# Ten middle token tiles of an attention and two-stage MoE kernel, written out instead of looped over

## The chip, the cores and the metric

The kernel runs on one core of one Trainium2 chip. The metric is the device time of one execution in microseconds, lower is better.

## What is computed

Three stages follow each other, all in float32. Cut to what matters:

```python
def _attn_ref(q, k, v):                        # 8 batches, 8 heads, 576 tokens, head size 64
    scores = scale * np.matmul(q_c, k_c.transpose(0, 1, 2, 4, 3))   # within chunks of 64 tokens
    attn = np.exp(scores - scores.max(-1)); attn /= attn.sum(-1) + 1e-09
    out = np.matmul(attn, v_c)
def _moe_ref(x, w_in, w_out, s, b):            # x 4608 x 512, hidden 2048
    r = np.maximum(x @ w_in, 0.0)
    g = s * (r * r) + b
    return g @ w_out
def _moe2_ref(x, w_skip, w_gate, w1, w2):      # 8 experts, hidden 1024, one expert per token
    do_compute = x @ w_skip > 0
    e_idx = np.argmax(xc @ w_gate, axis=1)     # xc = x[do_compute]
    h = np.maximum(xc[mask] @ w1[e], 0.0)      # mask: e_idx == e
    y[mask] = gate_w[mask, None] * (h @ w2[e])
    out[do_compute] = xc + y
```

## The kernel before, in words

**Tiles.** The 4608 tokens are cut into 12 tiles of 384 tokens (`TILES`, `TOK`), a tile into 6 attention chunks of 64 tokens (`CPT`). The hidden layer of the first MoE is cut into 16 slices of 128 (`FT`). Every float32 product is made of three products of high and low parts (`_hi`, `_lo`).

**Two phases.** The first 960 us or so go over the 12 tiles: while TensorE does the first MoE of tile i, all engines also do the attention of tile i+1 and the routing of tile i-1. Then come the experts, in blocks of 128 gathered rows, in loops whose bounds are known only at run time.

**What a tile is on TensorE** (`tile`, L756 to L780): for each of the 16 slices f, `into_h` of slice f+1 (L714, matmuls on L723, 12 of 384 columns) and then `into_x2` of slice f (L728, matmuls on L738, 9 of 512 columns); between them stand the attention stages of tile i+1 that `stages(f)` names (L688, L695, L704) and, in slice 14, `rank` of the tile before (L749 to L753). The last slice calls `into_h(i + 1, 0, ...)`, so the first slice of the next tile is computed before the tile ends. That call waits for `x_ready`, which VectorE gives on L1140 when the last attention chunk is in. At the end of a tile TensorE waits for `route_step` (L778).

**The other engines** have a `tile` of the same shape. ScalarE (L997): `relu` (L985), square (L989), the high part of g (L916) and its share of the attention. VectorE (L1253): the low part of g (L1186), `keep_x2` of the tile before at slice 0 (L1196), the gate's dot products (L1207), `route_a` and `route_b` (L1246 to L1251 are its last steps, which need `rank`). GpSimd (L580): low parts of q, k and v and, behind each tile, `send_records` (L563). SyncE loads and stores in a loop of its own, one tile an iteration (L451).

**What sets the order.** The order is written out by hand, in the sequence of calls on each engine; engines meet at counting semaphores. Tile 0 and tile 11 are straight code (L807, L811). Tiles 1 to 10 are a loop of five iterations with two tiles in each, on TensorE (L808), ScalarE (L1028), VectorE (L1296) and GpSimd (L607). The two tiles of an iteration differ in the buffer z (1, then 0). Inside the loop the tile's number is held in a register, so a wait for a count such as `CPT * i + end // CHUNK` is preceded by register operations; in straight code it is a constant. An iteration's end is a compare-and-branch back to its start. TensorE's is:

```python
            tile(0, 0, True, False)
            with pe.Fori(0, (TILES - 2) // 2) as two:
                tile(two * 2 + 1, 1, True, True)
                tile(two * 2 + 2, 0, True, True)
            tile(TILES - 1, 1, False, True)
```

Of the kernel before, what the change touches and what calls it, by code (L numbers as in the profile page):

```python
# [17 lines left out]
def chunked_attention_moe(nc, first_qk_rows, first_v_rows, qk, v, w_in, w_out, moe_s, moe_b, gate_rows, gate_cols_in, w1, w2, out):  # L18
    CHUNK = 64
    D = 64  # L20
    N, DM = out.shape
    FF = w_in.shape[0] * w_in.shape[2] // (DM // P)
    E, _, F = w1.shape
    KT = DM // P
    FT = FF // P
# [4 lines left out]
    TILES = N // TOK  # L30
# [41 lines left out]
    with ctx:  # L72
# [244 lines left out]
        def stages(f):  # L317

            found = []
            for c in range(CPT):  # L320
                for name, at in (("D", 2 * c + 4), ("C", 2 * c + 3), ("B", 2 * c + 1), ("A", max(2 * c - 1, 0))):
                    if at == f:
                        found.append((name, c))
            return found
# [192 lines left out]
        def _(pool):  # L517
# [23 lines left out]
            def lo_of_qk(n, c):  # L541

                pool.wait_ge(qk_hi, n - CPT + 1)
                pool.tensor_tensor(qk_rest[:, :], qk_raw[:, c % SLOTS, :], qk_top[:, :].bitcast(F32),  # L544
                                   ALU.subtract).then_inc(qk_split, 1)

            def lo_of_v(n):

                pool.wait_ge(v_hi_done, n - CPT + 1)
                pool.tensor_tensor(v_lo[:, :], v_raw[:, :], v_hi[:, :].bitcast(F32), ALU.subtract).then_inc(v_split, 1)  # L550
# [7 lines left out]
            def send_records(i):  # L558

                pool.wait_ge(table_clear, 16)  # L560
                pool.wait_ge(records_ready, i + 1)
                for t in range(SUB):
                    pool.indirect_dma_start(  # L563
                        out=table[:, :], out_offset=bass.IndirectOffsetOnAxis(ap=slot[:, t:t + 1].bitcast(U32), axis=0),
                        in_=record[:, t, :], in_offset=None, bounds_check=E * REGION - 1,
                        oob_is_err=False).then_inc(records_out, 16)
# [13 lines left out]
            def tile(i):  # L580
                for f in range(1, FT):
                    for stage, c in stages(f - 1):
                        if stage == "A":
                            lo_of_qk(CPT * (i + 1) + c, c)
                        if stage == "C":
                            lo_of_v(CPT * (i + 1) + c)
                    if isinstance(i, int) and i == 0 and f % 2 and f + 2 < JOBS:
                        column_sums(f + 2)
# [15 lines left out]
                    split_half(step - 2)  # L604
            column_sums(1)
            tile(0)
            with pool.Fori(1, TILES - 1, 2) as odd:  # L607
                for i in (odd, odd + 1):
                    tile(i)
                    send_records(i - 1)  # L610
            def gather(count, stored):

                pool.wait_ge(x2_stored, 32 * stored)
# [33 lines left out]
        def _(pe):  # L647
# [108 lines left out]
            def tile(i, z, attend, route):  # L756

                for f in range(FT):
                    if attend and f == 2 * CPT + 2:
                        into_h(i, f + 1, z, range(1))  # L760
                        attention("D", CPT * (i + 1) + CPT - 1, CPT - 1)
                        into_h(i, f + 1, z, range(1, KT))
                    elif f + 1 < FT:
                        into_h(i, f + 1, z, begin=0 if route or f > 0 else FIRST_PART)
                    elif attend:
                        into_h(i + 1, 0, 1 - z)
                    if route and f == RANK_AT[attend]:
                        if attend:
                            pe.wait_ge(probs_kept, CPT * (i + 1) + CPT)
                        rank(i - 1)  # L770
                    if attend and f != 2 * CPT + 2:
                        for stage, c in stages(f):
                            attention(stage, CPT * (i + 1) + c, c)
                    if not route and f == FT - 1:
                        column_sums()
                    into_x2(i, f)
                if route and attend:
                    pe.wait_ge(route_step, ROUTE_STEPS * (i - 1) + RANKS_READ)  # L778
                if not route:
                    pe.wait_ge(bias_done, 1)  # L780

            def column_sums():

                pe.wait_ge(column_step, JOBS - 1)
                pe.wait_ge(exp_done, 2 * CPT)
                pe.matmul(s_ps[:, :], products[:, 0:P], bias[:, :], start=True, stop=True).then_inc(sums_done, 1)
# [18 lines left out]
            into_h(0, 1, 0, range(KT // 2, KT), end=FIRST_PART)  # L805
            into_h(0, 0, 0, begin=FIRST_PART)
            tile(0, 0, True, False)  # L807
            with pe.Fori(0, (TILES - 2) // 2) as two:  # L808
                tile(two * 2 + 1, 1, True, True)
                tile(two * 2 + 2, 0, True, True)  # L810
            tile(TILES - 1, 1, False, True)  # L811

            ht_ps = [s_ps, av_ps]
# [100 lines left out]
        def _(act):  # L914
# [82 lines left out]
            def tile(i, z, attend, route):  # L997
                for f in range(FT):
                    relu(i, f)
                    waiting = stages(f - 1) if attend and f > 0 else []  # L1000
                    order = {1: "AgCDB", FT - 1: "DgCAB"}.get(f, "CgADB")
                    for name in order:
                        if name == "g":
                            hi_of_g(i, f)
                        for stage, c in waiting:
                            if stage == name:
                                attention(stage, CPT * (i + 1) + c, c, 1 - z, i + 1)
                    if route and f == RANK_AT[attend]:
                        route_exp(i - 1)
                    if not route and EARLY + f < JOBS:  # L1010
                        split(EARLY + f)
                    for e, j in jobs_at(f) if not attend else ():
                        split2(e, 1 - e, j)
# [11 lines left out]
            act.wait_ge(scalars_in, 32)  # L1025
            act.wait_ge(sums_done, 1)
            act.activation(bias[:, :], s_ps[:, :], ACT.Identity, scale=b_col[:, 0:1]).then_inc(bias_done, 1)
            with act.Fori(0, (TILES - 2) // 2) as two:  # L1028
                tile(two * 2 + 1, 1, True, True)
                tile(two * 2 + 2, 0, True, True)  # L1030
            tile(TILES - 1, 1, False, True)
            ht_ps = [s_ps, av_ps]

# [77 lines left out]
        def _(dve):  # L1111
# [141 lines left out]
            def tile(i, z, attend, route):  # L1253
                for f in range(FT):
                    waiting = stages(f - 1) if attend and f > 0 else []
                    order = "DCBg" if f == FT - 1 else "CBgD"
                    for name in order:
                        if name == "g":
                            lo_of_g(i, f)
                        for stage, c in waiting:  # L1260
                            if stage == name:
                                attention(stage, CPT * (i + 1) + c, c, 1 - z)
                    if route and f == 0:
                        keep_x2(i - 1)
                    if route and f < RANK_AT[attend]:
                        dots(i - 1, DOTS_BY[attend][f], DOTS_BY[attend][f + 1])
                    for stage, c in waiting:
                        if stage == "B":
                            attention("B2", CPT * (i + 1) + c, c, 1 - z)
                    if route and f == RANK_AT[attend] - 1:  # L1270
                        route_a(i - 1)
                    if route and f == RANK_AT[attend]:
                        route_b(i - 1)
                    if not attend and f == RANK_AT[attend]:
                        dve.wait_ge(route_step, ROUTE_STEPS * i)
                        for e in range(SOON):
                            es = next_row[:, e:e + 1]
                            dve.tensor_scalar(es, es, float(e * REGION + P), None, ALU.max).then_inc(first_closed, 1)
                        dve.wait_ge(first_closed, SOON)
                    if not route and EARLY + f < JOBS:  # L1280
                        split(EARLY + f)
                    for e, j in jobs_at(f) if not attend else ():
                        split2(e, 1 - e, j)
                    if not attend and f == FT - 4:
                        dve.wait_ge(got_in, 16)
                        dve.tensor_copy(idx[:, :], got[:, :]).then_inc(rows_held, 16)
# [6 lines left out]
            tile(0, 0, True, False)  # L1293
            dve.wait_ge(bias_done, 1)
            dve.wait_ge(gate_in, 16)
            with dve.Fori(0, (TILES - 2) // 2) as two:  # L1296
                tile(two * 2 + 1, 1, True, True)
                tile(two * 2 + 2, 0, True, True)
            tile(TILES - 1, 1, False, True)
            keep_x2(TILES - 1)  # L1300

# [181 lines left out]
```

## Time and profile before

| | |
|---|---|
| median of 3 runs | 1352.35 us (1352.3 to 1354.8) |
| the profiled execution's own time | 1355.16 us |
| its span in the trace | 1353.4 us |
| mean granted TensorE clock | 0.997 of full speed |
| instructions with a busy time | 22395 |

The profiled execution lies 2.8 us above the median, and its span is 1.8 us shorter than its own time. Times in the trace count from the first instruction of the span. PE is TensorE's matmuls, PEld its weight loads, DVE VectorE, ACT ScalarE, POOL GpSimd; a name ending in q (PEldq, DVEq) is that engine's sequencer, whose instructions are not counted as busy. "Idle before" is time in which the engine had nothing running, with what ended it; "issue" means that the profile shows nothing that it waited for.

### The profile page before, as it was taken

To read this page: it belongs to the slowest core of one execution; us is meant where nothing else is said; L and a number is where in the kernel's file an instruction comes from. 1 tells how busy PE (TensorE), PEld (TensorE's weight loads), DVE (VectorE), ACT (ScalarE), POOL (GpSimd) and SP (SyncE) were. 2 spreads that over 40 slices of the span, in tenths; PEclk is the share of its full clock that TensorE was granted. 3 is DMA by queue.
4 is the path that set the end of the run, shared out by engine and by line. 5 is a ranking of instruction groups with operands and counts; after the bars stand their busy time and mean duration, and the time that the engine had idled before them with its cause. 6 is when DMAs were issued, how large, how long until landed. Compare 5 with 4: busy or idle time off the path is not lost.

```text
span 1353.4 us, 22395 instructions
## 1 busy us (share of the span) xinstructions
PE 1329.0 (98%) x7066; PEld 1171.8 (87%) x7067; DVE 927.9 (69%) x2141; ACT 753.0 (56%) x1838; POOL 311.1 (23%) x274
## 2 busy tenths in 40 slices
PE   8999999999999999999999999999998999999998
PEld 7998999899998999889998999988786778888886
DVE  3887869688786978778796878867548673333232
ACT  4886757576674757567575766646346552222221
POOL 4642223121322212221322222101111111111111
PEclk9999999999999999999999999999899999999999
DMA  7531202031121302112030302044618641111110
GB/s 261 171 116 58 98 29 98 22 103 39 44 93 30 100 30 99 32 50 88 32 106 22 106 24 91 23 141 127 218 59 296 226 146 47 39 47 39 46 38 27
DMA packets 61589, 116.95 MB, mean 86 GB/s; under 512 B 11848, under 2 KB 20296, under 8 KB 61360
## 3 DMA queue, kind: packets, MB, share of 16 engines
q1 hardware_dynamic: 44496, 81.11, 18.0%
q10 hardware_dynamic: 10880, 20.97, 4.4%
q0 software_dynamic: 6112, 13.56, 3.2%
q8 instruction: 58, 0.95, 0.3%
q14 instruction: 43, 0.35, 0.1%
HBM read 91.28 MB, written 27.08 MB: 87 GB/s over the span
## 4 chain that ended last, share of the span: by engine, by line
PE 90%; DVE 5%; issue 3%; ACT 1%; DVEq 1%; POOLq 0%; POOL 0%; ACTq 0%
PE h_ps L723 29%; PE y_ps L738 28%; PE y_ps L848 10%; PE h_ps L834 10%; PE s_ps L688 3%; PE av_ps L704 3%; DVE weights_lo L1180 2%; PE t_ps L695 1%; PE s_ps L842 1%; PE t_ps L820 1%; PE av_ps L842 1%; PE h_ps L651 0%; DVE rows_t_lo L1313 0%; DVE weights_lo L1171 0%; DVE g_lo L1186 0%
## 5 line engine op out<-in xcount | busy, mean ns | idle before, releaser
L1207 DVE CUSTOM_DVE_ANT_0 products<-scratch,wide 128x512 f32<-128x512 f32 x297 | 287.3, 967 | 6.7
L723 PE MATMUL h_ps<-rows_t_hi,weights_lo 128*128 128x384 f32 (+2 forms) x776 | 262.1, 338 | 7.8 <-issue 5.6
L723 PE MATMUL h_ps<-rows_t_hi,weights_hi 128*128 128x384 f32 (+2 forms) x776 | 260.9, 336 | 0.0
L723 PE MATMUL h_ps<-rows_t_lo,weights_hi 128*128 128x384 f32 (+2 forms) x776 | 259.7, 335 | 0.0
L985 ACT ACTIVATE scratch<-h_ps 128x384 f32<-128x384 f32 x192 | 94.5, 492 | 294.5 <-PE h_ps L723 289.8
L738 PE MATMUL y_ps<-weights_hi,g_lo 128*128 128x512 f32 x576 | 228.1, 396 | 1.6 <-DVE g_lo L1186 1.6
L738 PE MATMUL y_ps<-weights_lo,g_hi 128*128 128x512 f32 x576 | 226.5, 393 | 0.0
L738 PE MATMUL y_ps<-weights_hi,g_hi 128*128 128x512 f32 x576 | 225.9, 392 | 0.0
L1186 DVE TENSOR_TENSOR g_lo<-scratch,g_hi 128x384 fp32r<-128x384 f32 x192 | 120.1, 626 | 91.7 <-ACT g_hi L916 89.2
L723 PEld LDWEIGHTS h_ps<-rows_t_hi,weights_lo 128*128 128x128 f32 x776 | 145.8, 188 | 21.5 <-issue 7.3
L544 POOL TENSOR_TENSOR qk_lo<-qk_raw,qk_hi 128x768 fp32r<-128x768 f32 x66 | 125.3, 1899 | 141.6 <-ACT qk_hi L916 141.6
L723 PEld LDWEIGHTS h_ps<-rows_t_lo,weights_hi 128*128 128x128 f32 x776 | 145.8, 188 | 7.0
L550 POOL TENSOR_TENSOR v_lo<-v_raw,v_hi 128x256 fp32r<-128x256 f32 x66 | 49.1, 744 | 436.3 <-ACT v_hi L916 436.3
L723 PEld LDWEIGHTS h_ps<-rows_t_hi,weights_hi 128*128 128x128 f32 x776 | 145.6, 188 | 0.0
L738 PEld LDWEIGHTS y_ps<-weights_hi,g_hi 128*128 128x128 f32 x576 | 108.1, 188 | 23.7
L738 PEld LDWEIGHTS y_ps<-weights_hi,g_lo 128*128 128x128 f32 x576 | 108.2, 188 | 20.5 <-DVE g_lo L1186 2.7
L738 PEld LDWEIGHTS y_ps<-weights_lo,g_hi 128*128 128x128 f32 x576 | 108.2, 188 | 17.0 <-issue 0.2
L933 ACT ACTIVATE soft<-s_ps,row_bias 64x64 f32<-64x64 f32 x528 | 120.4, 303 | 3.0
L916 ACT ACTIVATE rows_t_hi<-av_ps 64x256 fp32r<-64x256 f32 (+2 forms) x165 | 68.2, 413 | 67.5 <-PE av_ps L842 58.9
L916 ACT ACTIVATE g_hi<-scratch 128x384 fp32r<-128x384 f32 x192 | 100.8, 525 | 6.1
L848 PE MATMUL y_ps<-weights_hi,rows_t_lo 128*128 128x512 f32 x240 | 97.2, 405 | 6.1 <-DVE rows_t_lo L1313 5.7
L834 PE MATMUL h_ps<-weights_hi,rows_t_lo 128*128 128x512 f32 x244 | 102.1, 418 | 0.0
(178 smaller groups left out, 2377.1 us busy)
## 6 DMA issues: line engine op xcount, KB each, us to landing
qk_raw<-in_qk SPq DMA_DIRECT2D x66, 384.0 KB, 3.0
expert_raw<-in_w ACTq DMA_DIRECT2D x25, 512.0 KB, 5.4
expert_raw<-in_w SPq DMA_DIRECT2D x21, 512.0 KB, 5.4
out<-scratch SPq DMA_DIRECT2D x12, 768.0 KB
x_rows<-scratch SPq DMA_DIRECT2D x12, 768.0 KB
v_raw<-in_v SPq DMA_DIRECT2D x66, 128.0 KB, 2.0
scratch<-in_w ACTq DMA_DIRECT2D x15, 512.0 KB
wide<-in_w_out SPq DMA_DIRECT2D x7, 512.0 KB, 4.5
```

The source lines that it names most:

```text
L544: pool.tensor_tensor(qk_rest[:, :], qk_raw[:, c % SLOTS, :], qk_top[:, :].bitcast(F32), ALU.subtract).then_inc(qk_split, 1)
L550: pool.tensor_tensor(v_lo[:, :], v_raw[:, :], v_hi[:, :].bitcast(F32), ALU.subtract).then_inc(v_split, 1)
L688: mm = pe.matmul(s_ps[:, J * 256:(J + 1) * 256], qt[:, J, :], kt[:, J, :], start=m == 0, stop=m == 2)
L723: mm = pe.matmul(h_ps[f % 2][:, begin:end], w[:, f // PAIR, kt, fs], x[:, z, kt, begin:end], start=kt == 0 and n == 0, stop=kt == KT - 1 a ...
L738: mm = pe.matmul(y_ps[t][:, :], g[:, f % 2, ts], w[:, f, :], start=f == 0 and n == 0, stop=f == FT - 1 and n == 2)
L834: mm = pe.matmul(h_ps[f][:, :], x[:, kt, :], w[par][:, f, kt, :], start=kt == 0 and n == 0, stop=kt == KT - 1 and n == 2)
L848: mm = pe.matmul(y_ps[0][:, :], h[:, t, :], w[par][:, t, :], start=t == 0 and n == 0, stop=t == ET - 1 and n == 2)
L916: return act.activation(out_, in_, ACT.Copy)
L933: last = act.activation(probs[xs, c % 2, h, :], s_blocks[xs, h, x, :], ACT.Exp, bias=row_bias[xs, h:h + 1], scale=SCALE)
L985: act.activation(r_buf[f % 2], h_ps[f % 2][:, 0:TOK], ACT.Relu).then_inc(r_done, 1)
L1186: dve.tensor_tensor(GL[:, f % 2, :], u_buf[f % 2], GH[:, f % 2, :].bitcast(F32), ALU.subtract).then_inc(g_ready, 1)
L1207: dve.tensor_tensor_reduce(products[:, :], x2_sb[:, t, :], gate_w[:, e, :], 1.0, 0.0, ALU.mult, ALU.add, logits[:, t, e:e + 1]).then_inc(d ...
```

## The change

On TensorE, ScalarE, VectorE and GpSimd the loop over pairs of tiles is replaced by a Python loop, which writes tiles 1 to 10 out one behind the other. The tile's number is then a constant in every wait. SyncE's loop over tiles, the work of a tile and its order are as before.

```diff
@@ GpSimd, L607 @@
             tile(0)
-            with pool.Fori(1, TILES - 1, 2) as odd:
-                for i in (odd, odd + 1):
-                    tile(i)
-                    send_records(i - 1)
+            for i in range(1, TILES - 1):
+                tile(i)
+                send_records(i - 1)
@@ TensorE L808; the same edit on ScalarE L1028 and VectorE L1296 @@
             tile(0, 0, True, False)
-            with pe.Fori(0, (TILES - 2) // 2) as two:
-                tile(two * 2 + 1, 1, True, True)
-                tile(two * 2 + 2, 0, True, True)
+            for i in range(1, TILES - 1):
+                tile(i, i % 2, True, True)
             tile(TILES - 1, 1, False, True)
```

## Rows read from the trace of the kernel before

**Rows 1.** The page: busy time by engine, and the chain that ended last.
```profile
PE 1329.0 (98%) x7066; PEld 1171.8 (87%) x7067; DVE 927.9 (69%) x2141; ACT 753.0 (56%) x1838; POOL 311.1 (23%) x274
...
PE 90%; DVE 5%; issue 3%; ACT 1%; DVEq 1%; POOLq 0%; POOL 0%; ACTq 0%
```

**Rows 2.** Waits, 109 to 891 us: waiter <- awaited: total us, times, longest.
```profile
PEld h_ps L723 <- issue: 7.3, 4, 2.3
...
PE h_ps L723 <- issue: 5.6, 4, 1.9
PE h_ps L723 <- DVE rows_t_lo L1140: 1.7, 5, 0.3
```

**Rows 3.** Stretches, one a tile (1, 2, 3, 4, 6, 8, 10): us, busy, clock, DMA.
```profile
109.19:186.44 77.25, 77.25 (x430) 70.34 (x430) 63.16 (x152) 50.87 (x140) 19.20 (x15) 1.00 0.19 62
186.44:265.19 78.75, 77.22 (x430) 70.13 (x429) 63.76 (x154) 50.32 (x139) 18.71 (x15) 1.00 0.19 62
265.19:342.64 77.45, 77.45 (x430) 70.71 (x431) 61.40 (x150) 50.31 (x139) 18.71 (x15) 1.00 0.19 62
342.64:421.56 78.92, 77.24 (x430) 70.15 (x429) 63.89 (x154) 50.31 (x139) 18.71 (x15) 1.00 0.19 61
...
499.01:578.54 79.53, 77.26 (x429) 70.17 (x429) 64.48 (x155) 50.32 (x139) 18.71 (x15) 1.00 0.19 61
...
656.00:734.69 78.69, 77.22 (x430) 70.13 (x429) 63.67 (x154) 50.32 (x139) 18.71 (x15) 1.00 0.19 61
...
812.11:889.67 77.56, 77.23 (x430) 70.47 (x430) 62.57 (x152) 50.32 (x139) 18.72 (x15) 1.00 0.15 50
sum 780.48, PE 773.18 PEld 704.21 DVE 626.30 ACT 503.70 POOL 187.58; mean PE 77.32 PEld 70.42 DVE 62.63 ACT 50.37 POOL 18.76
```

**Rows 4.** The chain, 255 to 275 us: start us, us, what.
```profile
259.55 2.35 PE h_ps L723 x12
261.90 2.09 PE y_ps L738 x9
263.99 1.21 issue
265.19 2.32 PE h_ps L723 x12
```

**Rows 5.** The chain, 184 to 190 us and 882 to 895 us.
```profile
186.44 2.10 PE h_ps L723 x12
...
889.67 2.10 PE h_ps L723 x12
```

**Rows 6.** Branches of loops, by line: ns min/median/max.
```profile
L808 PEldq COMPARE_BRANCH  x5: 83/4738/5475, 260.3 to 886.0; - x5
...
L1296 DVEq COMPARE_BRANCH  x5: 60/68/72, 259.2 to 884.9; - x5
...
L900 PEldq COMPARE_BRANCH  x20: 67/208/214, 1060.0 to 1332.3; - x20
```

**Rows 7.** DMA queues, 109 to 891 us, then 260.5 to 266.5 us: packets, MB.
```profile
q8 instruction: 43, 0.70, 0.5%
...
q8 instruction: 2, 0.03, 4.6%
```

**Rows 8.** Timeline, PE and DVE, tiles 1, 2 and 11: rank's end, next step.
```profile
179.63 0.22 PE L753 MATMUL t_ps<-chosen,ones 128*128 128x8 bf16 x3
...
179.96 0.18 DVE L1246 TENSOR_TENSOR place<-t_ps,next_row 128x24 f32<-128x24 f32 x1 [1.44 <-PE t_ps L753]
...
256.85 0.22 PE L753 MATMUL t_ps<-chosen,ones 128*128 128x8 bf16 x3
...
257.52 0.18 DVE L1246 TENSOR_TENSOR place<-t_ps,next_row 128x24 f32<-128x24 f32 x1 [1.80 <-PE t_ps L753]
...
929.47 0.22 PE L753 MATMUL t_ps<-chosen,ones 128*128 128x8 bf16 x3
...
929.79 0.18 DVE L1246 TENSOR_TENSOR place<-t_ps,next_row 128x24 f32<-128x24 f32 x1 [1.51 <-PE t_ps L753]
```

**Rows 9.** Timeline, DVE, first work behind the loop's end, tile 3.
```profile
263.58 0.56 DVE L1186 TENSOR_TENSOR g_lo<-scratch,g_hi 128x384 fp32r<-128x384 f32 x1 [3.49 <-ACT g_hi L916]
264.17 1.41 DVE L1196 SCALAR_TENSOR_TENSOR scratch<-y_ps,s_col,bias 128x512 f32<-128x512 f32 x2
```

More of the change, by code:

```diff
@@ L1027, in _ @@
             act.activation(bias[:, :], s_ps[:, :], ACT.Identity, scale=b_col[:, 0:1]).then_inc(bias_done, 1)
-            with act.Fori(0, (TILES - 2) // 2) as two:
-                tile(two * 2 + 1, 1, True, True)
-                tile(two * 2 + 2, 0, True, True)
+            for i in range(1, TILES - 1):
+                tile(i, i % 2, True, True)
             tile(TILES - 1, 1, False, True)
@@ L1295, in _ @@
             dve.wait_ge(gate_in, 16)
-            with dve.Fori(0, (TILES - 2) // 2) as two:
-                tile(two * 2 + 1, 1, True, True)
-                tile(two * 2 + 2, 0, True, True)
+            for i in range(1, TILES - 1):
+                tile(i, i % 2, True, True)
             tile(TILES - 1, 1, False, True)
```

## The prediction

> **What bounds the kernel now.** Read the page first: TensorE's matmuls are busy for 1329.0 us, 98% of the span, and the chain that ended last runs on PE for 90% of it [rows 1]. With no matmul taken away, a change can win only what PE is idle or late, so the next view is the waits of PE in the part that the change touches, 109 to 891 us. What PE waited for there is short to tell: four times "issue", 5.6 us in all, which is PE waiting for nothing that another engine owes it, and five times VectorE's L1140, 1.7 us; the weight loads show the same four stops as 7.3 us [rows 2]. Four is the number of jumps back in a loop of five iterations, five is the number of second tiles.
>
> Then the stretches: I cut the loop at the start of each tile's `into_h(i, 1)`, which gives a duration per tile [rows 3]. The first tile of a pair takes 77.25 us (tile 1) or 77.45 us (tile 3), the second 78.69 to 79.53 us when a jump back follows and 77.56 us in tile 10, where none does. The granted clock is 1.00 in all of them. So the cost is at a place, not spread.
>
> The chain shows that place: behind the 9 matmuls of the last slice (261.90 us) come 1.21 us of issue, then `into_h(3, 1)` at 265.19 us, whose 12 matmuls take 2.32 us [rows 4]. The same 12 at the boundary inside a pair take 2.10 us and follow without a gap, as they do at the loop's exit [rows 5]: same work, no jump. The sequencer's own rows name the cause: TensorE's branch on L808 has a median of 4.7 us and a maximum of 5.5 us, and a minimum of 83 ns, the one not taken [rows 6]. It is issued some 3.7 us ahead of the last matmul (from 260.3 us, against an end at 263.99 us), which is why only part of it shows. Between 260.5 and 266.5 us the queue that carries instructions moved two blocks of 16 KB, where 43 in 782 us is the mean of one in 18 us [rows 7]: I read it as fetching the loop's start anew. The loops of the expert phase jump in 0.2 us [rows 6], so it is not a jump as such, but a jump to code that is no longer held.
>
> **The change, part by part.** All durations are of the profiled execution (1355.16 us, span 1353.4); it is 2.8 us above the median of 1352.35. The terms are differences inside it, and I take them off the median.
>
> *The four jumps back on TensorE go.* Ends of second tiles: 78.75 + 78.92 + 79.53 + 78.69 = 315.89 us, against 4 x 77.56 = 310.24 us of the tile without a jump: 5.65 us. The first matmuls behind a jump refill the pipeline (2.32 against 2.10 us), which stands in the odd tiles: all ten sum to 780.48 us, the even ones to 315.89 + 77.56 = 393.45, the odd ones to 387.03, against 5 x 77.25 = 386.25: 0.78 us. Together **6.43 us**. This sum agrees with the 5.6 us of waits and 4 x 0.2 of refill.
>
> *The late step of VectorE in second tiles.* The second tile without a jump (77.56) is 0.31 us longer than the first (77.25). The timeline says where: in tile 1 `rank` ends at 179.63 + 0.22 = 179.85 us and VectorE's L1246 starts 0.11 us later; in tile 2 it ends at 257.07 and L1246 starts 0.45 us later; in tile 11, which is straight code, 0.10 us later [rows 8]. Behind L1246 stand L1140 and `x_ready`, for which PE's `into_h(i + 1, 0)` waits; that is the 1.7 us in five times [rows 2]. The code of both tiles is the same but for constants and the register arithmetic, so the 0.34 us is tied to the position in the instruction stream or to the registers; written out, neither is repeated five times at that spot. I take 5 x 0.31 = **1.55 us**. Bounds: nothing, if it comes back at other tiles' L1246, or 1.55 us lost more (ten times instead of five).
>
> *Register operations before waits go* on all four engines. On PE they stand beside matmuls that run anyway: in tiles 1 and 3 the PE is busy for the whole stretch, 77.25 of 77.25 and 77.45 of 77.45 us [rows 3]. On VectorE and ScalarE they could shorten the path to `x_ready`: the 12 matmuls behind it take 2.35 us in tile 2 [rows 4] against 2.10, so at most about 0.25 us in each of 10 tiles, 2.5 us, could be won. I take 0, because L1246 to L1251 are paced by their own results, and keep the 2.5 us for the low end.
>
> *The jumps on VectorE, ScalarE and GpSimd go.* VectorE's takes 0.07 us [rows 6] and its next work is 3.49 us later, waiting for ScalarE's g_hi [rows 9]; GpSimd is busy 23% of the span. Worth 0: ScalarE's own jump is hidden by the same wait for PE's h.
>
> *What is late next, where the stall goes.* PE will ask for `into_x2(3, 0)` 1.2 us earlier, and that needs g_lo and the y banks that `keep_x2` frees from 264.17 us on, 1.41 us for two of them [rows 9]. Without the stall `into_h(3, 1)` ends at 263.99 + 2.10 = 266.1 us, g_lo is done at 264.14 and the second bank at 265.58 (for 266.1 + 0.7). The cover holds, by at least 1 us, and the boundary inside a pair has the same order with no gap. SyncE's loop is not changed; DMA is at 0.19 in these stretches, and its loads follow PE's progress.
>
> *The longer code.* The number of executed instructions falls a little, so the fetches of 16 KB stay about 43 less the extra ones. In straight sequence they cost PE nothing: of 43 fetches between 109 and 891 us only those at the four jumps have a wait beside them [rows 2, 7]. The nearest row for a fetch that would not be hidden is the jump's 1.2 to 1.9 us.
>
> Sum: 6.43 + 1.55 = 7.98 us, all on the path that sets the end. What follows (tile 11 and the experts) is the same code started earlier: 1352.35 - 8.0 = **1344.4 us**, 0.6% faster.
>
> One page of the Trainium skill speaks against this. "Advanced Engine Details and Errata", section Control Flow Timing, gives a compare-and-branch about 108 ns; by that figure four jumps would be worth an estimated 0.4 us and nothing would be measured. The branches that are not taken or short agree with it (83 ns and 68 ns), the 4.7 us of L808 do not, and the measurement decides.
>
> **The rivals.**
> - *The late step stays or moves* (chance 0.15). Only the jumps' 6.43 us go: 1345.9 us. If L1246 is late in all ten tiles, 1.55 us more are lost: 1347.5 us. For it: the cause of the 0.34 us is not in any row. Against: tile 11.
> - *The jump was not the cause, the boundary is* (0.03). If PE needs a refill of instructions at this point whatever stands there, the four stops stay, and the time is within 1 us of 1352.35. Against: two kinds of boundary without jump and without gap [rows 5].
> - *Fetches fall behind in straight code: slower* (0.03). TensorE's ten tiles become some 35 blocks never run before, where each must arrive in its turn. The place is PE's wait "issue" in mid-tile. It decides from 8.0 / 35 = 0.23 us a block; at the 0.5 us that would be a part of the jump's stop, it is 35 x 0.5 - 8.0 = 9.5 us slower, 1361.9 us. Against: tiles 0 and 11 and 30-odd blocks inside the loop show none.
> - *A loop of the experts loses its quick jump* (0.05). Their code moves to other addresses. If a jump of 0.2 us on L900 becomes one of 4.7, hidden for the most part as at L808, it costs about 1.4 us each time; once or twice, 1345.8 to 1347.2 us; in all 20, 28 us, which would be slower by 20. For the latter nothing speaks: these loops are short.
>
> **How the numbers follow.** The forecast has 0.74. A difference of under 0.2%, 2.7 us, can't be told from no change in this kernel, so "faster" means under 1349.6 us. Forecast, late step and most of the experts' case lie below it: 0.94. No change 0.03, slower 0.03. The range: from 1344.4 less the 2.5 us of the register operations, 1341.9, a little lower for the runs' scatter, to 1347.5 of the first rival and a little more: 1341.5 to 1348.5 us.
>
> **What would show it.** In the profile after: no wait "PE h_ps <- issue"; ten stretches of about 77.25 us, summing to about 772.5 instead of 780.5; no branch on TensorE before the experts; L1246 0.10 us behind `rank` in each tile; no cluster of 16 KB blocks at the former jumps. Wrong would be: a new PE wait in mid-tile, a second tile still 0.3 us longer (first rival), or an expert phase (from the first matmul of L834 on) that takes longer than before.

## The result and the profile after

The change makes the kernel faster by 0.7%: 1346.04 us (median of 5, 1345.08 to 1346.25) against 1353.69 us of the kernel before on the same chips (median of 5), ratio 0.9934 with a 95% interval of 0.991 to 0.9958. The forecast was 1344.4 us within 1341.5 to 1348.5.

The page of the kernel after, busy times and the queues that carry instructions:

```profile
span 1344.0 us, 21173 instructions
...
PE 1327.1 (99%) x7066; PEld 1172.1 (87%) x7067; DVE 929.0 (69%) x2141; ACT 753.1 (56%) x1838; POOL 311.1 (23%) x274
...
q8 instruction: 49, 0.80, 0.3%
```

Not a matmul more or less (7066), and PE is busy for 1327 of 1344 us. The 22395 instructions of before and the 21173 of after count the sequencers' own too; with a busy time there are 18386 in both. The sequencers execute 1449 register operations and branches less and 227 semaphore instructions more.

The stretches, cut at the same points of the program as [rows 3], tiles 1, 2, 3, 10 and the sum of ten:

```profile
108.58:186.00 77.42, 77.42 (x431) 70.43 (x430) 63.26 (x152) 50.84 (x140) 19.22 (x15) 1.00 0.20 62
186.00:263.22 77.22, 77.22 (x432) 70.51 (x430) 62.60 (x152) 50.27 (x139) 18.70 (x15) 1.00 0.20 62
263.22:340.44 77.22, 77.22 (x430) 70.50 (x430) 62.56 (x152) 50.25 (x139) 18.70 (x15) 1.00 0.20 62
...
803.63:880.83 77.20, 77.20 (x431) 70.49 (x430) 62.59 (x152) 50.27 (x139) 18.71 (x15) 1.00 0.15 50
sum 772.25, PE 772.25 PEld 704.82 DVE 626.47 ACT 503.23 POOL 187.51; mean PE 77.22 PEld 70.48 DVE 62.65 ACT 50.32 POOL 18.75
```

In the kernel before, even tiles took 78.7 to 79.5 us and tile 10 77.56 [rows 3]. Now first and second tiles of a pair are alike at 77.2 us (tile 1 took 77.4), and in the whole sum PE is busy for 772.25 of 772.25 us. The ten tiles are 780.48 - 772.25 = 8.23 us shorter; 7.98 was forecast.

The waits in the same stretch; those of PE on "issue" and on L1140 [rows 2] are gone. Of PEld's the long ones on "issue" are gone; left are the one for `x_ready` (L1137 is L1140 of before) and short ones that stood there before too:

```profile
PEld h_ps L722 <- DVE rows_t_lo L1137: 4.0, 10, 0.4
...
PEld t_ps L748 <- issue: 1.6, 10, 0.2
```

The chain at the end of tile 2, where 1.21 us of issue stood [rows 4]:

```profile
261.13 2.08 PE y_ps L737 x9
263.21 2.10 PE h_ps L722 x12
```

And VectorE behind `rank` in tile 2: `rank` ends at 256.42 + 0.22 = 256.64, the next step starts 0.10 us later, not 0.45 us [rows 8].

```profile
256.42 0.22 PE L752 MATMUL t_ps<-chosen,ones 128*128 128x8 bf16 x3
...
256.74 0.18 DVE L1243 TENSOR_TENSOR place<-t_ps,next_row 128x24 f32<-128x24 f32 x1 [1.55 <-PE t_ps L752]
```

The span fell by 9.4 us, 1.2 more than the ten tiles. Of that, 0.6 us lie ahead of tile 1 and 0.8 in tile 11, whose code did not change (the experts took 0.2 us more). Tile 11 differs from execution to execution: here are tile 11 and the experts of the kernel before, and tile 11 of the kernel with only TensorE written out.

```profile
889.51:962.06 72.55, 71.28 (x375) 63.92 (x373) 50.62 (x115) 38.60 (x64) 7.46 (x7) 0.99 0.54 175
962.06:1353.40 391.34, 379.75 (x1822) 309.06 (x1822) 180.18 (x390) 134.42 (x202) 63.98 (x62) 0.99 0.28 97
```

```profile
882.30:953.85 71.55, 70.28 (x374) 62.96 (x373) 50.59 (x115) 38.60 (x64) 7.46 (x7) 1.00 0.53 174
```

The last three columns are granted clock, DMA share and GB/s. At a clock of 1.00 tile 11 takes 71.55 us, and 72.55 at 0.99; the changed kernel run once more took 73.07 us there at 0.98. The clock is not all of it: in `mid_jump` below it took 73.41 us at 1.00, with 1.7 us of waits for g_lo. So **the sum over the ten tiles is the measure used below**: for the changed kernel it repeated within 0.15 us (772.25 and 772.39), while whole executions scatter by some microseconds. Some executions also reach tile 1 about 7.6 us later (116.2 instead of 108.6 us), such as the profiled ones of `one_jump` and `pad40`, which is why their spans (1356.0 and 1357.3 us) are long and their tiles are not.

### The profile page after: what moved, and what is told of

It is laid out like the page before. It is cut to its first block, busy times and chain, and to the rows that moved or that the text cites. A ratio compares the mean times of both kernels' runs of the same rounds, so it can differ in the third digit from the quotient of the medians.

```text
span 1344.0 us, 21173 instructions
## 1 busy us (share of the span) xinstructions
PE 1327.1 (99%) x7066; PEld 1172.1 (87%) x7067; DVE 929.0 (69%) x2141; ACT 753.1 (56%) x1838; POOL 311.1 (23%) x274
## 4 chain that ended last, share of the span: by engine, by line
PE 91%; DVE 4%; issue 2%; ACT 1%; DVEq 1%; POOLq 0%; POOL 0%; ACTq 0%
PE h_ps L722 29%; PE y_ps L737 29%; PE y_ps L846 11%; PE h_ps L832 10%; PE s_ps L687 3%; PE av_ps L703 3%; DVE weights_lo L1177 2%; PE t_ps L694 1%; PE s_ps L840 1%; PE t_ps L818 1%; PE av_ps L840 1%; PE h_ps L650 0%; DVE weights_lo L1168 0%; DVE rows_t_lo L1309 0%; DVE g_lo L1183 0%
## 5 line engine op out<-in xcount | busy, mean ns | idle before, releaser
L722 PE MATMUL h_ps<-rows_t_hi,weights_hi 128*128 128x384 f32 (+2 forms) x776 | 261.2, 337 | 0.0
```

What stands on the lines that cost most here:

```text
L722: mm = pe.matmul(h_ps[f % 2][:, begin:end], w[:, f // PAIR, kt, fs], x[:, z, kt, begin:end], start=kt == 0 and n == 0, stop=kt == KT - 1 a ...
```

## The experiments

Medians and ratios are against runs of the kernel before on the same chip; "ten tiles" is from the first matmul of tile 1's `into_h(1, 1)` to that of tile 11, in one trace of each kernel (780.49 us before, 772.25 after).

### pe_only, pe_looped and dve_only: which engine's loop

`pe_only` is the kernel before with the edit on TensorE alone; `dve_only` the same on VectorE alone; `pe_looped` is the changed kernel with this put back:

```diff
-            for i in range(1, TILES - 1):
-                tile(i, i % 2, True, True)
+            with pe.Fori(0, (TILES - 2) // 2) as two:
+                tile(two * 2 + 1, 1, True, True)
+                tile(two * 2 + 2, 0, True, True)
```

> The kernel before with TensorE's loop alone written out; VectorE, ScalarE and GpSimd keep theirs. Theory (TensorE's four jumps back to code no longer held cost 6.4 us, VectorE's late step 1.6 us): about 6.4 us faster than before, 1347 us against 1353.7; the ten tiles sum to about 774 us, the second tiles of a pair 0.3 us longer than the first, VectorE's step behind rank late by 0.46 us in them. Rival (the loops of the other engines hold TensorE up at the pair's end, as VectorE's sequencer too is stopped for some 3 us behind its jump): under 3 us faster, and waits of TensorE for another engine at the pair's end.

> The changed kernel with TensorE's loop put back; the other three engines stay written out. Theory: 6.4 us slower than the changed kernel and 1.6 us faster than before, about 1352 us; four waits of 1.2 to 1.9 us on TensorE, no late step on VectorE. Rival (other engines' loops matter): 4 us or more faster than before.

> The kernel before with VectorE's loop alone written out. Theory: about 1.6 us faster than before, all of it in second tiles, where the step behind rank comes 0.11 us behind it as in first tiles. Rival (the late step is made by TensorE's, ScalarE's or GpSimd's side): the step stays 0.46 us late in second tiles and the time is that of before.

| kernel | median us | ratio to before (95%) | ten tiles us |
|---|---|---|---|
| pe_only | 1346.61 | 0.9949 (0.9935 to 0.9962) | 774.03 |
| pe_looped | 1351.71 | 0.9982 (0.9973 to 0.9992) | 778.31 |
| dve_only | 1350.96 | 0.9966 (0.9944 to 0.9989) | 779.02 |

`pe_only` takes 6.46 us off the ten tiles; 6.43 was the term. Its PE waits in the ten tiles are one row:

```profile
PE h_ps L723 <- DVE rows_t_lo L1139: 1.7, 5, 0.3
```

The late step is still there, 0.46 us in every second tile, and the stops at the jumps are gone although the three other engines still loop. So no other engine's loop holds TensorE up. `dve_only` is the mirror: the step is 0.11 us behind `rank` in all ten tiles, the jumps' stops are there in full, and the ten tiles are 1.47 us shorter (1.55 was the term):

```profile
PE h_ps L723 <- issue: 5.9, 4, 1.8
```

`pe_looped` has the four stops (4.9 us of issue) and no late step: 6.06 us more than the changed kernel in the ten tiles, 2.2 us less than before. The two parts add up, 6.46 + 1.47 = 7.93 of 8.24 us. How exact that is, the stops tell: the same four jumps stopped PE for 5.64 us before, 5.89 in `dve_only` and 4.91 in `pe_looped`, so a sum of ten tiles with the jumps in it scatters by up to a microsecond. With each kernel's own stops taken out, the late step is worth 1.7 us by `dve_only`, 1.5 by `pe_looped` and 1.8 by the changed kernel against `pe_only`. In the medians `dve_only` came out 2.6 us better than before, more than its tiles show; the scatter of whole executions covers the difference.

### short_jumps and sizes: is it the jump or what it jumps to

`short_jumps` adds ten jumps back to the changed kernel:

```diff
             for i in range(1, TILES - 1):
                 tile(i, i % 2, True, True)
+                with pe.Fori(0, 2):
+                    pe.wait_ge(cleared, 2)
```

> The changed kernel with a loop of two rounds over one wait, long satisfied, behind each of the ten middle tiles on TensorE: ten jumps back of a few instructions. Theory (only a jump to code that is no longer held costs): same time as the changed kernel within 0.5 us, TensorE without a gap at the tile's end. Rival (any jump empties the sequencer's supply): ten gaps of 1.2 us or more, 12 us slower than the changed kernel.

1346.17 us, ratio 0.9945 (0.9928 to 0.9962), ten tiles 772.27 us against 772.25: ten jumps cost nothing that can be seen. PE has no wait at all in the ten tiles. A taken one of these branches takes 0.21 us (the maximum 228 ns) and one not taken 76 ns.

`sizes` puts loops of different length ahead of everything; `probe(n)` is n matmuls of 128 columns:

```diff
             warm(5)
+            with pe.Fori(0, 3):
+                probe(100)
...
+            with pe.Fori(0, 3):
+                probe(1100)
```

> The changed kernel with six loops of three rounds on TensorE in front of everything, of 100, 300, 500, 700, 900 and 1100 small matmuls (a matmul is two instructions, so some 200, 600, 1000, 1400, 1800 and 2200). The added matmuls write a bank that nobody reads, so the time itself, some 0.5 to 1 ms longer, says nothing. Theory: the branch of short bodies takes about 0.2 us and that of long ones 4 us or more, with the change between 1000 and 2200 instructions, since the loop of two tiles has about 1800 and costs. Rival (the cost has nothing to do with the body's length): all six branches take about the same.

The branches of the loops with 500, 700, 900 and 1100 matmuls, min/median/max in ns of three, the last of them not taken:

```profile
L797 PEldq COMPARE_BRANCH  x3: 76/208/208, 363.0 to 576.3; - x3
...
L799 PEldq COMPARE_BRANCH  x3: 76/208/208, 725.7 to 1024.3; - x3
...
L801 PEldq COMPARE_BRANCH  x3: 76/3305/3342, 1216.3 to 1600.3; - x3
...
L803 PEldq COMPARE_BRANCH  x3: 76/3303/3643, 1835.0 to 2304.4; - x3
```

With 1400 instructions in the body the way back takes 0.2 us, with 1800 it takes 3.3 us, and 2200 cost the same as 1800 (3.3 and 3.6 us). The queue that carries TensorE's instructions says why. In the first line below it moves five blocks of 16 KB for all three rounds of the loop of 1400, all of them in the first round; in the second it moves 18 for rounds two and three of the loop of 1800, nine a round:

```profile
q8 instruction: 5, 0.08, 0.1%
...
q8 instruction: 18, 0.29, 0.3%
```

The loops of 200, 600 and 1000 fetch nothing in their third round either, and that of 2200 fetches eleven blocks a round. So the step lies between 1400 and 1800 instructions. The loop of two tiles executes 1816 an iteration and fetches nine blocks in each, in `mid_jump` too: it pays because its body is longer than what TensorE holds, and not because it jumps. I had expected 4 us or more; 3.3 was measured, with no other transfer under way. (The whole run took 3650 us, 2.3 ms longer and not the 0.5 to 1 ms expected, which changes nothing in the branches.)

The second reading of this run is as useful: PE has no idle time between 1024.5 and 2304 us. The small matmuls take 0.21 us each (a round of 900 takes 1408.3 - 1216.3 = 192.0 us), so those already queued outlast the branch. A branch of 3.3 us stops nobody here.

### one_jump and mid_jump: how many, and where

```diff
-            with pe.Fori(0, (TILES - 2) // 2) as two:
...
+            with pe.Fori(0, 2) as four:
+                for n in range(4):
+                    tile(four * 4 + n + 1, (n + 1) % 2, True, True)
+            tile(TILES - 3, 1, True, True)
+            tile(TILES - 2, 0, True, True)
```

> The kernel before with TensorE's loop as two iterations of four tiles and the last two tiles written out, so one jump back in place of four. Theory (each jump costs the same however long the body, since its target is fetched anew): three quarters of the jumps' cost go, 4.8 us faster than before, with one wait of 1.2 to 1.9 us behind tile 4. Rival (a longer way back costs more): the one wait is over 2.5 us.

1349.86 us, ratio 0.9964 (0.995 to 0.9977). Ten tiles 775.79 us, 4.7 us shorter than before as forecast and 1.76 us above `pe_only`: one jump, one stop of 1.8 us. Its branch took 5.3 us over a body twice as long, within the 4.7 to 5.5 us of the two-tile loop [rows 6]; a longer way back adds nothing that can be seen, as `sizes` says too.

`mid_jump` leaves the loop but moves its end away from the tile's end (`tile` gets two more arguments, its first slice and the one behind its last):

```diff
...
+            CUT = 2
+
+            def to_cut(i):
+                tile(i, 1, True, True, 0, CUT)
+                into_h(i, CUT + 1, 1)
...
+            def from_cut(i):
+                into_x2(i, CUT)
+                tile(i, 1, True, True, CUT + 1, FT)
+                tile(i + 1, 0, True, True)
+            to_cut(1)
+            with pe.Fori(0, (TILES - 2) // 2 - 1) as two:
+                from_cut(two * 2 + 1)
+                to_cut(two * 2 + 3)
+            from_cut(TILES - 3)
```

> The kernel before with TensorE's loop turned by two slices: its end lies in slice 2 of a first tile, behind into_h of slice 3 and ahead of the wait for g_ready, not at the end of a tile. Three jumps back over the same 1800 instructions. Theory (the branch takes 4.7 us wherever it stands, and what shows is what TensorE's queued work doesn't cover; at the tile's end the sequencer comes late, since it stood at the wait for x_ready): the branches still take 4.5 to 5.5 us and TensorE's stop behind them is under 0.5 us each, ten tiles 774 to 775.5 us, 5 to 6 us faster than before. Rival (a jump to code no longer held stops TensorE for 1.2 us or more wherever it stands): three stops of 1.2 us or more, ten tiles about 778.5 us, 1.6 to 2 us faster than before.

1349.33 us, ratio 0.9948 (0.9918 to 0.9978); ten tiles 776.12 us, the branch and the waits:

```profile
L822 PEldq COMPARE_BRANCH  x4: 83/3690/3893, 271.4 to 737.8; - x4
```

```profile
PE h_ps L723 <- DVE rows_t_lo L1155: 1.7, 5, 0.3
PE y_ps L738 <- issue: 1.3, 3, 0.6
```

Three jumps cost 776.12 - 774.03 = 2.1 us against `pe_only`, 0.7 us each, where at the tile's end they cost (780.49 - 774.03) / 4 = 1.6 us each. The place matters, but not for the theory's reason. The stops are 0.57, 0.37 and 0.33 us, ten tiles 776.1 and not 775.5 at most, and the branch took 3.7 to 3.9 us, not 4.5 or more. What TensorE's queued work covers, from the start of the branch to the end of the last matmul, is 3.52 us at each of the three jumps here and 3.66 to 3.71 us at each of the 21 jumps at a tile's end (in the kernel before, `pe_looped`, `dve_only`, `one_jump` and the two padded kernels below): it is no shorter at the tile's end. The whole gain of the place is a shorter branch.

The traces also show what makes it shorter. In all 28 slow branches one block of 16 KB is fetched: its packet starts 0.95 to 1.5 us behind the branch's start, and the branch ends 1.2 to 1.5 us behind the packet's end. The packet takes 0.9 to 1.3 us in `sizes` and in `mid_jump`, and 1.8 to 3.1 us at a tile's end, where queue 0 (GpSimd's records, some 95 packets) is at work at the same time and is not at the other two places. First the kernel before, 261.2 to 263.8 us (5.9% of 16 engines for 2.6 us are 2.4 us), then `mid_jump`, 427.5 to 429.5 us (1.3 us):

```profile
q8 instruction: 1, 0.02, 5.9%
...
q0 software_dynamic: 62, 0.00, 1.8%
```

```profile
q8 instruction: 1, 0.02, 4.0%
```

That queue 0 is what slows the packet is argued from this coincidence; no run takes it away alone.

### pad40 and pad128: what VectorE's late step is

```diff
+            for n in range(40):
+                dve.memset(pad[:, n:n + 1], 0.0)
             for step in range(CPT + 2):
```

> The kernel before with 40 tiny memsets ahead of VectorE's work (on a tile nobody reads, while it would wait for the first scores), so that all its later code lies 40 instructions further on. Theory (the late step hangs on where the instruction lies, a block's border of 8 KB): in second tiles the step behind rank is 0.11 us behind it, the second tiles are 0.3 us shorter, about 1.5 us faster than before. Rival (register arithmetic or the step's own waits): still 0.46 us, same time.

> As the run with 40, with 128 memsets: 128 instructions of 64 bytes are 8 KB, one whole block. Theory (border of a block): the late step is back at 0.46 us in second tiles and nowhere else. Rival (a place in the stream that is not periodic in 128): it is not there. The start may come some microseconds later because of the memsets.

Forty instructions further on, the step is 0.11 us behind `rank` in all ten tiles and tile 10 takes 77.20 us, not 77.56; ten tiles 778.55 us, 1.9 us shorter, with four stops at the jumps as before. The median is 1351.07 us, ratio 0.9974 (0.996 to 0.9989): nothing but a shift of the code, and faster. With 128, it is back, in the second tiles alone: `rank` (L754 here) ends at 256.25 + 0.22 = 256.47 and the step starts 0.46 us later.

```profile
256.93 0.18 DVE L1247 TENSOR_TENSOR place<-t_ps,next_row 128x24 f32<-128x24 f32 x1 [1.82 <-PE t_ps L754]
...
256.25 0.22 PE L754 MATMUL t_ps<-chosen,ones 128*128 128x8 bf16 x3
```

Its ten tiles take 780.74 us, those of before 780.49. The lateness therefore hangs on where the instruction lies, with a period that 128 instructions fit: the step comes 0.35 us later there, and it shows because at this spot VectorE has nothing else to do and TensorE waits for it. The traces tie it to a fetched block. In the kernel before, queue 14, which moves instructions in blocks of 8 KB, starts one 0.66 to 0.71 us behind the start of the late step in each of the five second tiles, and the same in `pad128`; behind the steps of first tiles and all those of `pad40` it starts none for 3 us. Here are 257.5 to 259.5 us of the kernel before:

```profile
q14 instruction: 1, 0.01, 1.1%
```

So the late step is the one at which VectorE goes on to another block; that these blocks are VectorE's is read from their moving with its code. The last step of this kind, behind tile 11, is late too in some kernels (0.42 us in `mid_jump`, 1.48 in `pad128`) without such a packet near it, which stays open. `pad128` and `sizes` were executed once each.

### x_before_route and route_last: what is left in a tile

The changed kernel still loses something at every tile: the weight load waits 0.4 us for `x_ready` and the 12 matmuls behind it refill the pipeline. On VectorE `x_ready` stands behind `route_b`, which waits for `rank`. Both kernels move `route_b` in the ten middle tiles; the first ahead of g_lo in slice 15, the second behind it. `x_before_route`:

```diff
                         if name == "g":
+                            if route and attend and f == FT - 1:
+                                route_b(i - 1)
                             lo_of_g(i, f)
...
-                    if route and f == RANK_AT[attend]:
+                    if route and not attend and f == RANK_AT[attend]:
                         route_b(i - 1)
```

`route_last` has the same last edit, and in place of the first, behind the loop over the names:

```diff
+                    if route and attend and f == FT - 1:
+                        route_b(i - 1)
```

> The changed kernel with VectorE's route_b of the ten middle tiles moved behind its last attention step (L1137) in slice 15, so that x_ready no longer waits for rank. Theory (each tile still loses 0.2 to 0.35 us at into_h of the next tile, for x_ready): tiles of 76.9 to 77.0 us instead of 77.2, 2 to 3 us faster than the changed kernel. Rival (g_lo of slice 15 now comes 1.1 us later and into_x2 waits for it, or the stop only moves to ScalarE's x_hi): no gain, or a new wait for g_lo.

1347.31 us against 1346.26 us of the changed kernel measured beside it, ten tiles 774.17 against 772.39: **slower by 0.18 us a tile**. The wait for `x_ready` shrank and another took its place:

```profile
PEld y_ps L737 <- DVE g_lo L1183: 4.8, 10, 0.5
PEld h_ps L722 <- DVE rows_t_lo L1137: 2.1, 11, 0.5
```

The rival held. In the changed kernel the first steps of `route_b` are done while VectorE waits for `rank`; here all of it, 1.95 us, stands between the last attention step and g_lo of slice 15. The changed kernel beside it:

> The changed kernel unchanged, on the same chip as the two others, for comparison: 0.9934 of before, ten tiles 772.3 us, tile 11 71.5 us.

It gave 1346.26 us, ratio 0.9912 (0.988 to 0.9944), against runs of the kernel before that scattered more (median 1357.66 us); the ratio of `mid_jump` is against the same runs. Its ten tiles and the 0.9934 of the first comparison are the better number; tile 11 took 73.07 us and not 71.5, at a clock of 0.98.

> The changed kernel with VectorE's route_b of the ten middle tiles moved behind both x_ready and g_lo of slice 15, the last work of the tile on VectorE. In the run that moved it behind x_ready alone the wait for x_ready was gone and a wait for g_lo had come, tiles 77.4 us instead of 77.2. Theory (both are needed before route_b's result is): neither wait, TensorE's first matmuls of the next tile without refill, tiles of 76.9 to 77.0 us, ten tiles 769.5 to 770.5 us, 2 us faster than the changed kernel. Rival (what remains is ScalarE's x_hi, which ends 0.9 us before x_ready can): tiles of 77.1 us or more.

Three tiles of it and the waits of its ten:

```profile
107.15:184.31 77.16, 77.16 (x430) 70.37 (x430) 63.22 (x152) 50.88 (x140) 17.29 (x13) 1.00 0.20 62
184.31:261.29 76.98, 76.98 (x431) 70.47 (x430) 62.51 (x152) 50.33 (x139) 18.78 (x16) 1.00 0.19 62
261.29:338.26 76.97, 76.97 (x431) 70.46 (x430) 62.49 (x152) 50.33 (x139) 18.82 (x15) 1.00 0.20 62
```

```profile
DVE rows_t_lo L1137 <- ACT rows_t_hi L914: 31.3, 10, 3.1
...
PEld h_ps L722 <- DVE rows_t_lo L1137: 1.6, 10, 0.2
```

Ten tiles 769.88 us, 2.4 us less than the changed kernel, and a median of 1343.53 us, 2.5 us below 1346.04. The ratio to before is 0.9939 (0.9917 to 0.996), no better than the changed kernel's 0.9934, since two of its eight executions took 1351.8 and 1352.0 us; it is the ten tiles that show the gain. The 12 matmuls behind the wait take 2.11 us in place of 2.33. VectorE now waits for ScalarE ahead of L1137, so `x_ready` comes as early as ScalarE allows, and `rank`'s followers come 3.4 us behind it, which costs TensorE nothing.

## Why the prediction was right

**The jumps, 6.43 us.** Right in place, cause and size: 6.46 us with TensorE alone written out, 6.06 us the other way round in `pe_looped`. The reading that it is the target that must be fetched, not the jump, was an inference from the 0.2 us of L900; `sizes` shows it in the blocks fetched, and sets it between 1400 and 1800 instructions. The branches to held code take 0.21 us taken and 0.08 us not taken. Beside that stands the figure of the Trainium skill ("Advanced Engine Details and Errata", section Control Flow Timing), about 108 ns for a compare-and-branch: the order of magnitude for these, and not for the 3.3 to 5.5 us of the others.

**The late step, 1.55 us.** Right in size (1.5 to 1.9 us by `dve_only`, `pe_looped` and `pad40`), and in that it would not come back: it is at 0.11 us in all tiles of the kernel after. The text left open whether place or register arithmetic makes it, and gave the two as equals. It is the place: `pad40` keeps all register operations and is rid of it. That it did not fall on another tile's critical step was luck of the layout as much as anything; in `pe_only`, `mid_jump` and both padded kernels the last `rank` step was late by 0.27 to 1.48 us.

**Register operations, 0 us.** Taken as nothing with up to 2.5 us as low end. Ten tiles give 8.24 us against 7.93 for the two parts; the 0.3 us between them is less than the stops scatter, so nothing can be seen of them. The 2.5 us were there to be had, but by an order of work (`route_last`), not by fewer register operations.

**The cover.** Said to hold by at least 1 us: PE has no wait for g_lo or the y banks in the ten tiles. The experts' quick jumps stayed quick (the 20 branches of their inner loop take 219 ns at most after the change), and their stretch took 391.5 us against 391.3.

**Straight code.** "Stay about 43 less the extra ones": 34 blocks moved between 108.6 and 880.8 us, nine less, against the "some 35" of the rival, and none of them stops PE. The slower rival's place, a wait on issue in mid-tile, is empty. One weight load waited 0.3 us on "issue" once.

**The total.** 8.0 us were taken off 1352.35, the median of the three runs shown; the five-run median of before is 1353.69 us, and the measured difference is 7.65 us. The forecast of 1344.4 is 1.6 us low; 1.3 us of it is the other median of before, and the rest is the 7.65 us against 7.98. That a forecast 0.3 us from the measured difference came out is in part luck, since a median moves by more than that: the ten tiles, 8.24 us, are what bears it out.

## What to carry to other kernels

Look at the branch rows of the sequencers before anything is written out: a loop that jumps in 0.2 us gains nothing from it, and one that takes microseconds costs only what the engine's queued work doesn't cover. Both are in the trace: the start of the branch, its duration, and the end of the last queued matmul. If such a loop has to stay, look at what else is transferred while it jumps, since that is what differed between the dear place and the cheap one here. Where two bodies of the same code differ by a third of a microsecond, ask where in the stream the step lies before asking what it computes. And a step whose result is needed late (here `route_b`) should not stand before one that the bounding engine waits for; but ask what else stands behind it, as the first attempt shows.

## What the runs showed of the hardware that I had not expected

- TensorE jumps back over 1400 instructions in 0.21 us without fetching any, and over 1800 in 3.3 us, fetching nine blocks of 16 KB in each round; there is no step between 200 and 1400.
- The same fetched jump took 3.3 to 3.6, 3.7 to 3.9 and 4.6 to 5.5 us at three places; most of the difference is the time of one packet of 16 KB, 0.9 to 1.3 us or 1.8 to 3.1 us.
- TensorE's queued matmuls covered 3.5 to 3.7 us of the branch at both places in a tile.
- Code moved by 40 instructions on VectorE, with nothing else changed but 40 small memsets ahead of it, is worth 1.9 us in the ten tiles, and 128 undo it.
